# Decay attention, MLP and gated convolution in one kernel: order of loads, weight casts and the mixed input xr

## The chip, the cores and the metric

The kernel runs on one core of a Trainium2 chip. The metric is device time in microseconds (us) of one launch. TensorE (PE) multiplies matrices, VectorE (DVE), ScalarE (ACT) and GpSimd (POOL) do the elementwise work, and the queue of SyncE (SP) issues the loads and stores. Each engine works through its own queue in the order in which it was written; semaphores tie the queues together.

## The reference

Two batches, 768 tokens, model width 512, MLP width 1024, all float32. Three parts follow each other.

```python
# 1. attention with decay, 8 heads of width 64, state carried from block to block
intra = (q k^T * Dmask) v;   inter = (q * lam_pow) kv_state
out = intra + inter;         kv_state = lam_block * kv_state + (k * rev_pow)^T v
# 2. MLP on x and the token before it
xk = mu_k * x + (1 - mu_k) * x_prev;   xr = mu_r * x + (1 - mu_r) * x_prev
k = maximum(xk @ w_k, 0);   v = k * k @ w_v;   r = sigmoid(xr @ w_r);   x = r * v
# 3. gated convolution, 5 taps
gate = sigmoid(sum over taps of conv_w[j] * x shifted by 4 - j)
y = (gate * (x @ w_val)) @ w_out
```

## The kernel before

**Attention** goes over 12 chunks of 128 tokens (NCH = 12, six for each batch), all heads of a chunk at once. For chunk n TensorE does `scores(n)`, `update(n)` (the new state's product, not for the last chunk of a batch), `inter(n)` (not for the first chunk of a batch) and `attend(n)`. `scores(n + 1)` stands in front of `update(n)`. VectorE weighs the scores with the decay mask (`weigh`, two operations of 512 columns, L460) and adds the state (`new_state`, L474 and L477). GpSimd makes `kdec`, `qd` and `faded`. ScalarE copies the result out of PSUM into x (`evacuate_x`, L297), and `inter(n)` and `attend(n)` wait for the eviction of chunk n - 1, since they reuse its two banks.

Before it, TensorE does 24 dummy products (L781, WARM; each is two instructions in the trace), and VectorE makes the decay masks and `om` = 1 - mu from the small tensor `prm` (L546 to L552).

**Loads.** SP issues them all, in one written order (L198 to L218): `prm`, chunks 0 to 3, then weights and chunks mixed. A chunk is two tiles of 512 KB, qk and kv; it goes to one of four buffers, so `load_chunk(n)` waits for `att_done` of chunk n - 4, and what stands behind it on SP waits too. A weight piece is one tile of 512 KB: four for w_k, two for w_r, four for w_v. The four pieces of w2 (w_val and w_out) are issued when the last hidden product is done, into the place of w_k.

**Splitting.** Every operand of the MLP and the projections is split into a high part, cast to fp32r by ScalarE (`high`, `mix_high`, `kk_high`, L303, L320, L330), and a low part, the subtraction of the high part from the original, on VectorE (`low`, `mix_low`, `kk_low`, L495, L490, L504) or, for w_r and w_v, on GpSimd (L275). A product of k tiles is then three matmuls for each (L638, L639, L640): high by high, high by low, low by high.

**The MLP** goes over three tiles of 512 tokens (NT = 3, t = 0, 1, 2). For a tile TensorE does eight hidden products (`hidden(t, n)`, 12 matmuls of 512 columns each), four of receptance (`receptance(t, m)`, 12 each) and four value products (`value(t, m)`, 24 each). After each hidden product ScalarE does the relu (L326), VectorE the square (L499), then both split kk. `mix_part` (ScalarE, L314) and `mix` (VectorE, L484) build xk and xr. In each tile xr is built between its own hidden products: on ScalarE and VectorE alike one of its four steps stands with every second hidden product, the last high and low behind product 7. xk of the next tile is built during receptance. `new_x2` (L509) multiplies value and sigmoid, and writes in place into x.

What the order rests on: `hidden(0, 0)` waits for all of xk, w_k, the evictions of all 12 chunks, the weighing and the last state; `receptance(t, 0)` waits for all four `xr_l` of its tile and for w_r; `value(t, 0)` waits for all eight `kk_l` and for w_v; `hidden(t + 1, n)` with n of 4 or more waits for `new_x2(t, n - 4)`.

After the three tiles follow `val`, the taps of the convolution on VectorE (48 operations, L523), the gates and `project`, with stores of 256 KB each.

## Time and profile before

| | |
|---|---|
| median of 3 runs | 307.41 us (306.47 to 308.93) |
| the profiled execution | 305.9 us, of it span 304.0 us |
| TensorE busy | 286.8 us (94%) |
| VectorE, ScalarE, GpSimd busy | 164.6, 118.8, 48.1 us |
| mean granted clock of TensorE | 0.983 |
| HBM read, written | 20.01 MB, 3.15 MB |

The span runs from the first to the last instruction; the rest of the time lies around it. All times below are us from the start of the span. Attention fills the span up to 53, the three tiles of the MLP lie between 53 and about 234, and the rest follows.

### The profile page before, as it was taken

The numbers are of one execution on the slowest core, as the hardware profiler recorded it, in microseconds if no ns is written. First come the engines' busy times: TensorE is split into PE (matmuls) and PEld (weight loads), VectorE is DVE, ScalarE is ACT, GpSimd is POOL, SyncE is SP. The second block draws the span as 40 slices with busy tenths as digits, with TensorE's granted clock in tenths as the row PEclk, the third lists the DMA queues.
The fourth block names the chain that finished last, engine by engine and source line by source line (L and its number), as shares of the span: only waits on it lengthen the run. The fifth ranks groups of instructions, "written<-read, shape, count | busy, mean of one in ns | idle before, by whom it ended". The sixth has DMA issues, their size and how long they took to land.

```text
span 304.0 us, 4295 instructions
## 1 busy us (share of the span) xinstructions
PE 286.8 (94%) x1772; PEld 232.6 (77%) x1772; DVE 164.6 (54%) x251; ACT 118.8 (39%) x197; POOL 48.1 (16%) x38
## 2 busy tenths in 40 slices
PE   8998698999699999996999999789999999999996
PEld 8877586787488878875888888568887888887885
DVE  6547895298442004765444676621996879714100
ACT  1017624755362104645510155644711711612221
POOL 1684799950000000000000000000000000000000
PEclk9999899999799999999999999979999999999999
DMA  7999993000000000000000000070000000110122
GB/s 274 378 412 409 410 375 110 2 0 3 0 0 0 2 0 0 0 2 0 0 0 2 0 1 0 15 263 2 0 0 2 0 0 0 71 69 0 69 106 104
DMA packets 7506, 23.42 MB, mean 77 GB/s; under 512 B 832, under 2 KB 1216, under 8 KB 7488
## 3 DMA queue, kind: packets, MB, share of 16 engines
q1 hardware_dynamic: 7488, 23.16, 20.1%
q8 instruction: 14, 0.23, 0.3%
q14 instruction: 4, 0.03, 0.0%
HBM read 20.01 MB, written 3.15 MB: 76 GB/s over the span
## 4 chain that ended last, share of the span: by engine, by line
PE 90%; DVE 4%; DMA 3%; ACT 2%; issue 1%
PE ps L638 27%; PE ps L640 26%; PE ps L639 26%; PE ps L654 3%; PE ps L703 3%; DMA qk<-in_qk 3%; PE ps L781 2%; PE ps L671 1%; PE ps L688 1%; DVE xk_f L484 1%; DVE kk_f L499 1%; DVE pT L460 1%; DVE xr_l L490 1%; ACT ring L326 1%; DVE kk_l L504 1%
## 5 line engine op out<-in xcount | busy, mean ns | idle before, releaser
L638 PE MATMUL ps<-xk_h,wk_h 128*128 128x512 f32 x96 | 38.1, 397 | 0.8 <-issue 0.8
L639 PE MATMUL ps<-xk_l,wk_h 128*128 128x512 f32 x96 | 38.1, 396 | 0.0
L640 PE MATMUL ps<-kk_h,wv_l 128*128 128x512 f32 x96 | 38.1, 396 | 0.0
L638 PE MATMUL ps<-kk_h,wv_h 128*128 128x512 f32 x96 | 38.1, 396 | 0.0
L640 PE MATMUL ps<-xk_h,wk_l 128*128 128x512 f32 x96 | 38.0, 396 | 0.0
L639 PE MATMUL ps<-kk_l,wv_h 128*128 128x512 f32 x96 | 38.0, 396 | 0.0
L523 DVE SCALAR_TENSOR_TENSOR gate<-x,prm,gate 128x512 f32<-128x512 f32 x48 | 32.6, 746 | 0.0
L343 ACT ACTIVATE gate<-x,prm 128x512 f32<-128x512 f32 x12 | 8.7, 725 | 54.1 <-DVE x L509 54.1
L638 PE MATMUL ps<-xr_h,wr_h 128*128 128x512 f32 x48 | 20.7, 430 | 7.8 <-DVE xr_l L490 7.8
L499 DVE SCALAR_TENSOR_TENSOR kk_f<-ps,ring 128x512 f32<-128x512 f32 x24 | 16.5, 689 | 18.8 <-ACT ring L326 18.8
L509 DVE TENSOR_TENSOR x<-ps,r 128x512 f32<-128x512 f32 x12 | 8.3, 691 | 33.0 <-PE ps L640 33.0
L326 ACT ACTIVATE ring<-ps 128x512 f32<-128x512 f32 x24 | 14.3, 597 | 27.1 <-PE ps L640 27.1
L638 PEld LDWEIGHTS ps<-xk_h,wk_h 128*128 128x128 f32 x96 | 18.1, 188 | 5.4 <-issue 1.1
L639 PEld LDWEIGHTS ps<-kk_l,wv_h 128*128 128x128 f32 x96 | 18.1, 188 | 4.4
L640 PEld LDWEIGHTS ps<-kk_h,wv_l 128*128 128x128 f32 x96 | 18.1, 188 | 4.4
L640 PEld LDWEIGHTS ps<-xk_h,wk_l 128*128 128x128 f32 x96 | 18.1, 188 | 4.4
L638 PEld LDWEIGHTS ps<-kk_h,wv_h 128*128 128x128 f32 x96 | 18.1, 188 | 4.4
L639 PEld LDWEIGHTS ps<-xk_l,wk_h 128*128 128x128 f32 x96 | 18.1, 188 | 4.4
L460 DVE TENSOR_TENSOR pT<-ps,dec 128x512 f32<-128x512 f32 x24 | 15.3, 683 | 10.3 <-PE ps L654 10.2
L640 PE MATMUL ps<-xr_h,wr_l 128*128 128x512 f32 x48 | 20.2, 421 | 0.0
L639 PE MATMUL ps<-xr_l,wr_h 128*128 128x512 f32 x48 | 20.2, 421 | 0.0
L640 PE MATMUL ps<-w_h,gl 128*128 128x512 f32 (+1 forms) x52 | 19.8, 380 | 0.0
(69 smaller groups left out, 525.1 us busy)
## 6 DMA issues: line engine op xcount, KB each, us to landing
qk<-in_qk SPq DMA_DIRECT2D x12, 512.0 KB, 7.0
kv<-in_kv SPq DMA_DIRECT2D x12, 512.0 KB, 7.9
out<-out_sb SPq DMA_DIRECT2D x11, 256.0 KB, 2.0
wk_raw<-in_w_k SPq DMA_DIRECT2D x4, 512.0 KB, 10.1
wv_raw<-in_w_v SPq DMA_DIRECT2D x4, 512.0 KB, 8.7
wr_raw<-in_w_r SPq DMA_DIRECT2D x2, 512.0 KB, 8.5
w_raw<-in_w_val SPq DMA_DIRECT2D x2, 512.0 KB, 4.5
w_raw<-in_w_out SPq DMA_DIRECT2D x2, 512.0 KB, 8.0
```

The source lines that it names most:

```text
L326: nc.scalar.activation(ring[:, n % 4, :], ps[:, bank_of("mlp", t, n), :], ACT.Relu).then_inc(relu_ready, 1)
L343: nc.scalar.activation(like(t, gate[t][:, k, :]), x_cols(t, k, HALO), ACT.Copy, scale=prm[:, col:col + 1]).then_inc(tap0, 1)
L460: nc.vector.tensor_tensor(pT[:, n % 2, row, :], ps_s[n % 2][row], dec[:, row * PAIRS:(row + 1) * PAIRS, :].rearrange("p a i -> p (a i)"), ...
L499: nc.vector.scalar_tensor_tensor(out=kk_f[:, n, :], in0=ps[:, bank_of("mlp", t, n), :], scalar=0.0, in1=ring[:, n % 4, :], op0=ALU.max, op ...
L509: nc.vector.tensor_tensor(x_cols(t, m, 1), like(t, ps[:, bank_of("mlp", t, FT + KT + m), :]), like(t, r[:, m, :]), ALU.mult).then_inc(x2_r ...
L523: nc.vector.scalar_tensor_tensor(out=like(t, gate[t][:, k, :]), in0=x_cols(t, k, HALO - j), scalar=prm[:, col:col + 1], in1=like(t, gate[t ...
L638: nc.tensor.matmul(to, left(0), right(0), start=(i == 0), stop=False)
L639: nc.tensor.matmul(to, left(0), right(1), start=False, stop=False)
L640: done = nc.tensor.matmul(to, left(1), right(0), start=False, stop=(i == last))
L654: last = nc.tensor.matmul(ps_s[n % 2][row][:, cols], qk[i][rows_of(row), 1, cols], qk[i][rows_of(row), 0, cols], start=True, stop=True)
L703: last = nc.tensor.matmul(place_of(row, a), kv[i][:, 1, h * D:(h + 1) * D], pT[:, n % 2, row, a * P:(a + 1) * P], start=(c == 0 and a % 2 ...
L781: nc.tensor.matmul(ps[:, 7, 0:P], warm[:, :], warm[:, :], start=True, stop=True)
```

## The change

- `WARM` is 12 instead of 24.
- `prm` is issued by ScalarE, as its first instruction, and no more by SP.
- On SP only w_k's first piece stands ahead of chunk 4; the other weights move behind later chunks, all four pieces of w_v behind the last chunk.
- ScalarE: each weight cast of the attention stage but the first stands behind a later eviction than before (`wk_h` 1 behind that of chunk 5, `wk_h` 2 behind 7, `wk_h` 3 behind 8, `wr_h` 0 and 1 behind 9 and 10), and `wk_h` 0 behind that of chunk 2 instead of 3; the mixes of xk move a little. w_v is cast (`high`) behind hidden products 4 to 7 of tile 0.
- VectorE subtracts w_r (`low`) in place of GpSimd, and its steps on w_k and xk stand with other chunks. GpSimd keeps w_v.
- xr: for tile 0 the parts and mixes stand behind the last chunk, the high and low parts with hidden products 0 to 3. For tiles 1 and 2 all of it stands behind the receptance of the tile before.
- TensorE asks for all evictions at `hidden(0, 4)` and for the last state at `hidden(0, 6)`, instead of both at `hidden(0, 0)`.

```diff
-WARM = 24
+WARM = 12
@@ SP
-            sp.dma_start(prm[:, :], prm_in).then_inc(prm_here, 16)
             for n in range(IN_BUFS):
                 load_chunk(n)
             load_weight(wk_raw, w_k, 0, wk_here)
+            load_chunk(4)
             load_weight(wk_raw, w_k, 1, wk_here)
-            load_chunk(4)
+            load_chunk(5)
+            load_chunk(6)
             load_weight(wk_raw, w_k, 2, wk_here)
-            load_chunk(5)
+            load_chunk(7)
+            load_chunk(8)
             load_weight(wk_raw, w_k, 3, wk_here)
-            load_chunk(6)
-            load_chunk(7)
+            load_chunk(9)
+            load_chunk(10)
             load_weight(wr_raw, w_r, 0, wr_here)
-            load_chunk(8)
+            load_chunk(11)
             load_weight(wr_raw, w_r, 1, wr_here)
...
+            for i in range(4):
+                load_weight(wv_raw, w_v, i, wv_here)
@@ GpSimd
-            for i in range(2):
-                low(wr, wr_raw, i, wr_hi, wr_lo)
@@ ScalarE
+            act.dma_start(prm[:, :], prm_in).then_inc(prm_here, 16)
...
             evacuate_x(2)
+            high(wk, wk_raw, 0, wk_here, wk_hi)
             evacuate_x(3)
...
+            evacuate_x(5)
             high(wk, wk_raw, 1, wk_here, wk_hi)
-            evacuate_x(5)
+            mix_high(0, 2, 0)
+            mix_high(0, 3, 0)
+            evacuate_x(6)
+            evacuate_x(7)
             high(wk, wk_raw, 2, wk_here, wk_hi)
-            evacuate_x(6)
+            evacuate_x(8)
             high(wk, wk_raw, 3, wk_here, wk_hi)
-            evacuate_x(7)
-            evacuate_x(8)
+            evacuate_x(9)
             high(wr, wr_raw, 0, wr_here, wr_hi)
-            evacuate_x(9)
+            evacuate_x(10)
             high(wr, wr_raw, 1, wr_here, wr_hi)
-            evacuate_x(10)
-            high(wv, wv_raw, 0, wv_here, wv_hi)
             evacuate_x(11)
-            for i in range(1, 4):
-                high(wv, wv_raw, i, wv_here, wv_hi)
+            for k in range(KT):
+                mix_part(0, k, 1)
             for t in range(NT):
                 for n in range(FT):
-                    if n % 2 == 0:
-                        mix_part(t, n // 2, 1)
+                    if t == 0 and n < KT:
+                        mix_high(t, n, 1)
                     relu(t, n)
                     if n > 0:
                         kk_high(t, n - 1)
-                    if n % 2 == 1:
-                        mix_high(t, n // 2, 1)
+                    if t == 0 and n >= KT:
+                        high(wv, wv_raw, n - KT, wv_here, wv_hi)
...
+                if t + 1 < NT:
+                    for k in range(KT):
+                        mix_part(t + 1, k, 1)
+                    for k in range(KT):
+                        mix_high(t + 1, k, 1)
@@ VectorE
+                if n == 3:
+                    low(wk, wk_raw, 0, wk_hi, wk_lo)
                 if n == 4:
-                    low(wk, wk_raw, 0, wk_hi, wk_lo)
                     mix(0, 0, 0)
                     mix(0, 1, 0)
                 if n == 5:
                     mix(0, 2, 0)
                     mix(0, 3, 0)
+                if n == 6:
+                    low(wk, wk_raw, 1, wk_hi, wk_lo)
+                if n == 7:
                     mix_low(0, 0, 0)
-                if n == 6:
                     mix_low(0, 1, 0)
+                if n == 8:
                     mix_low(0, 2, 0)
-                if n == 7:
                     mix_low(0, 3, 0)
-                    low(wk, wk_raw, 1, wk_hi, wk_lo)
-                if n == 8:
+                if n == 9:
                     low(wk, wk_raw, 2, wk_hi, wk_lo)
-                if n == 9:
+                if n == 10:
                     low(wk, wk_raw, 3, wk_hi, wk_lo)
+                if n == 11:
+                    low(wr, wr_raw, 0, wr_hi, wr_lo)
+            low(wr, wr_raw, 1, wr_hi, wr_lo)
+            for k in range(KT):
+                mix(0, k, 1)
             for t in range(NT):
                 for n in range(FT):
-                    if n % 2 == 0:
-                        mix(t, n // 2, 1)
                     square(t, n)
                     if n > 0:
                         kk_low(t, n - 1)
-                    if n % 2 == 1:
-                        mix_low(t, n // 2, 1)
+                    if t == 0 and n < KT:
+                        mix_low(t, n, 1)
...
+                if t + 1 < NT:
+                    for k in range(KT):
+                        mix(t + 1, k, 1)
+                    for k in range(KT):
+                        mix_low(t + 1, k, 1)
@@ TensorE, hidden(t, n)
-                        pe.wait_ge(x_ready, NCH)
                         pe.wait_ge(p_ready, 2 * NCH)
-                        pe.wait_ge(state_ready, updates(NCH - 1))
+                if t == 0 and n == 4:
+                    pe.wait_ge(x_ready, NCH)
+                if t == 0 and n == 6:
+                    pe.wait_ge(state_ready, updates(NCH - 1))
```

## Rows read from the trace of the kernel before

**Rows 1.** The page, chain that ended last: shares of the span by engine.

```profile
PE 90%; DVE 4%; DMA 3%; ACT 2%; issue 1%
```

**Rows 2.** Waits of PE: who waited for whom, total us, times, longest us.

```profile
PE ps L638 <- DVE xr_l L490: 7.8, 3, 2.6
```

**Rows 3.** Chain in order of time, around `receptance(0, 0)`: start us, us, what.

```profile
76.23 0.60 ACT ring L326
...
78.15 0.61 DVE xr_l L490
...
78.81 0.51 PE ps L638
```

**Rows 4.** Table by stretch: us, busy of each engine, PEclk, DMA share, GB/s.

```profile
34.00:40.00 6.00, 5.76 (x80) 5.02 (x80) 5.24 (x10) 2.57 (x4) 4.60 (x4) 0.72 1.02 404
...
78.81:91.69 12.88, 12.88 (x48) 10.26 (x49) 5.33 (x8) 5.36 (x10) 0.00 (x0) 0.87 0.00 0
139.45:150.79 11.34, 11.34 (x49) 9.14 (x49) 5.33 (x8) 5.36 (x10) 0.00 (x0) 1.00 0.00 0
198.54:211.39 12.85, 12.85 (x48) 10.28 (x49) 2.77 (x4) 4.96 (x10) 0.00 (x0) 0.87 0.39 138
```

**Rows 5.** Timeline of ACT, 32 to 34: start us, us, what [idle before <-releaser].

```profile
32.57 1.04 ACT L303 CAST wk_h<-wk_raw 128x1024 fp32r<-128x1024 f32 x1
33.52 0.58 ACT L297 COPY x<-ps 128x512 f32<-128x512 f32 x1
```

**Rows 6.** Timeline of PE, from `attend(6)` to the first hidden product.

```profile
34.24 1.09 PE L703 MATMUL ps<-pT,kv 128*64 128x128 f32 x16 [2.64 <-ACT x L297]
35.27 2.08 PE L654 MATMUL ps<-qk 64*128 64x128 f32 x16
...
43.42 1.16 PE L654 MATMUL ps<-qk 64*128 64x128 f32 x16
...
46.74 1.16 PE L654 MATMUL ps<-qk 64*128 64x128 f32 x16
...
50.93 0.67 PE L688 MATMUL ps<-qd,state 64*64 64x128 f32 x16 [0.78 <-ACT x L297]
...
53.47 0.48 PE L638 MATMUL ps<-xk_h,wk_h 128*128 128x512 f32 x1 [0.85 <-issue]
```

**Rows 7.** Timelines of PE, ACT and DVE, the first 12 us.

```profile
1.05 7.27 PE L781 MATMUL ps<-warm 128*128 128x128 f32 x48 [1.05 <-DVE warm L540]
...
0.73 1.28 ACT L377 ACT_TABLE_LOAD   x1 [0.73 <-PEq L845]
...
6.58 0.96 DVE L552 TENSOR_SCALAR om<-prm 128x8 f32<-128x8 f32 x1
9.56 2.48 DVE L460 TENSOR_TENSOR pT<-ps,dec 128x512 f32<-128x512 f32 x4 [2.02 <-PE ps L654]
```

**Rows 8.** SP's issues of qk 1, 4, 11; under each, size and us to landing.

```profile
2.11 0.43 SPq L192 DMA_DIRECT2D qk<-in_qk  x1
qk<-in_qk SPq DMA_DIRECT2D x1, 512.0 KB, 5.7
...
12.13 0.33 SPq L192 DMA_DIRECT2D qk<-in_qk  x1
qk<-in_qk SPq DMA_DIRECT2D x1, 512.0 KB, 7.2
...
40.20 0.33 SPq L192 DMA_DIRECT2D qk<-in_qk  x1
qk<-in_qk SPq DMA_DIRECT2D x1, 512.0 KB, 4.8
```

**Rows 9.** Hidden products of tile 0: POOL and mix by line; one `kk_l` on DVE's timeline.

```profile
L275 POOL TENSOR_TENSOR wv_l<-wv_raw,wv_h 128x1024 fp32r<-128x1024 f32 x4 | 10.4, 2633 | 0.0
...
L484 DVE SCALAR_TENSOR_TENSOR xr_f<-x,om,xr_f 128x512 f32<-128x512 f32 x4 | 3.0, 745 | 7.0 <-ACT xr_f L314 7.0
...
60.60 2.08 DVE L504 TENSOR_TENSOR kk_l<-kk_f,kk_h 128x512 fp32r<-128x512 f32 x1
```

More of the change, by code:

```diff
@@ L201, in _ @@
             load_weight(wk_raw, w_k, 0, wk_here)
+            load_chunk(4)
             load_weight(wk_raw, w_k, 1, wk_here)
-            load_chunk(4)
+            load_chunk(5)
+            load_chunk(6)
             load_weight(wk_raw, w_k, 2, wk_here)
-            load_chunk(5)
+            load_chunk(7)
+            load_chunk(8)
             load_weight(wk_raw, w_k, 3, wk_here)
-            load_chunk(6)
-            load_chunk(7)
+            load_chunk(9)
+            load_chunk(10)
             load_weight(wr_raw, w_r, 0, wr_here)
-            load_chunk(8)
+            load_chunk(11)
             load_weight(wr_raw, w_r, 1, wr_here)
-            load_chunk(9)
-            load_weight(wv_raw, w_v, 0, wv_here)
-            load_chunk(10)
-            load_weight(wv_raw, w_v, 1, wv_here)
-            load_chunk(11)
-            load_weight(wv_raw, w_v, 2, wv_here)
-            load_weight(wv_raw, w_v, 3, wv_here)
+            for i in range(4):
+                load_weight(wv_raw, w_v, i, wv_here)
             sp.wait_ge(h_done, FT * NT)
@@ L380, in _ @@
             evacuate_x(2)
+            high(wk, wk_raw, 0, wk_here, wk_hi)
             evacuate_x(3)
-            act.wait_ge(om_ok, 1)
-            high(wk, wk_raw, 0, wk_here, wk_hi)
-            for k in range(KT):
+            for k in range(3):
                 mix_part(0, k, 0)
             evacuate_x(4)
-            for k in range(KT):
-                mix_high(0, k, 0)
-            high(wk, wk_raw, 1, wk_here, wk_hi)
-            evacuate_x(5)
-            high(wk, wk_raw, 2, wk_here, wk_hi)
-            evacuate_x(6)
-            high(wk, wk_raw, 3, wk_here, wk_hi)
-            evacuate_x(7)
-            evacuate_x(8)
-            high(wr, wr_raw, 0, wr_here, wr_hi)
-            evacuate_x(9)
-            high(wr, wr_raw, 1, wr_here, wr_hi)
-            evacuate_x(10)
-            high(wv, wv_raw, 0, wv_here, wv_hi)
-            evacuate_x(11)
-            for i in range(1, 4):
-                high(wv, wv_raw, i, wv_here, wv_hi)
+            mix_part(0, 3, 0)
+            mix_high(0, 0, 0)
+            mix_high(0, 1, 0)
+            evacuate_x(5)
+            high(wk, wk_raw, 1, wk_here, wk_hi)
+            mix_high(0, 2, 0)
+            mix_high(0, 3, 0)
+            evacuate_x(6)
+            evacuate_x(7)
+            high(wk, wk_raw, 2, wk_here, wk_hi)
+            evacuate_x(8)
+            high(wk, wk_raw, 3, wk_here, wk_hi)
+            evacuate_x(9)
+            high(wr, wr_raw, 0, wr_here, wr_hi)
+            evacuate_x(10)
+            high(wr, wr_raw, 1, wr_here, wr_hi)
+            evacuate_x(11)
+            for k in range(KT):
+                mix_part(0, k, 1)
             for t in range(NT):
                 for n in range(FT):
-                    if n % 2 == 0:
-                        mix_part(t, n // 2, 1)
+                    if t == 0 and n < KT:
+                        mix_high(t, n, 1)
                     relu(t, n)
```

## Prediction

> **What bounds the kernel now.** I began with the chain of work that ended last: TensorE holds 90% of it [rows 1], so a change pays where it closes a gap of TensorE, or where its clock was low. The table of waits names the gaps: three of 2.6 us in front of `receptance(t, 0)`, one for each tile t, all ending with `xr_l` from VectorE [rows 2]. The fourth gap of that size, 2.64 us, is in the attention stage and ends with ScalarE's eviction of x [rows 6]. The chain around the first kind shows why it is there [rows 3]: hidden products end at 76.2, and only then come relu (76.23), square, `kk_l`, and the last `xr_l`, which stands behind them in VectorE's order; the products with xr start at 78.81. The reader is to see that nothing in xr depends on the relu: only the order of the queue puts it there. The table of stretches adds the clock: the 48 receptance products take 12.88 and 12.85 us for tiles 0 and 2 (granted clock 0.87), and 11.34 for tile 1 (clock 1.00) after the same gap [rows 4]. In the attention stage ScalarE's queue explains the other gap: `wk_h` (L303) at 32.57 stands in front of the eviction at 33.52 [rows 5], and `attend(6)` waits for it until 34.24; the next scores then take 2.08 us where later ones take 1.16 [rows 6]. The clock of 34 to 40 is 0.72 [rows 4]. Loads run at full share and 404 GB/s meanwhile (last columns of that row): attention is close to a second bound, the DMA engines.
>
> **The attention stage, step by step.**
> *Start.* TensorE's 48 dummy matmuls take 7.27 us from 1.05 [rows 7]. Without half of them the row ends near 4.7 by the mean, later if the first ones are slow. `scores(0)` takes 1.1, then `scores(1)` waits for chunk 1's qk: it was issued at 2.11 and took 5.7, so 7.8 [rows 8]; with `prm` (0.43 us of SP's time, 84 KB) off SP's queue about 7.4. So dummies could end as late as 6.3 and cost nothing; that needs the removed 24 to be worth 2 us, 83 ns each, where the mean is 151. VectorE is the other input: its constants end at 6.58 + 0.96 = 7.54, yet it began to weigh at 9.56, held by scores [rows 7]. Now it weighs chunk 0 from 7.6 to 8.8; TensorE does scores(1) to 8.5, the update (0.6) to 9.1, attends (1.03) to 10.15. Before, attend(0) ended at 12.08. The start is 1.9 us earlier.
> `prm` is issued by ScalarE. If its table load of 1.28 us (0.73 [rows 7]) goes first, the constants and attend(0) are up to 1.3 late; if not, nothing. I take nothing, since the start has slack against the loads below.
> *Pace.* Without a wait a chunk takes 3.32 us: 43.42 to 46.74 [rows 6] (scores 1.09, update 0.61, inter 0.60, attend 1.03). Chunks 5 and 6 lack one part each, 2.7. Loads go in the order of the SP queue: chunk 4's qk is the 11th tile of 512 KB and landed at 12.13 + 7.2 = 19.33, chunk 11's qk the 31st, landed at 40.20 + 4.8 = 45.0 [rows 8]. That is 1.284 us per tile. The new order makes the qk of chunks 4 to 11 tiles number 10, 13, 15, 18, 20, 23, 25 and 28. From 18.9 for tile 11 (0.43 less) they land at 17.6, 21.5, 24.0, 27.9, 30.5, 34.3, 36.9, 40.7. Scores of the next chunk go in front of each attend, so attend(n) ends at the later of attend(n-1) and the landing of qk n+1, plus the chunk's time: 10.15, 13.5, 16.8, 20.9, 24.8, 27.55, 30.6, 34.0, 37.6, 41.0, 44.3. The waits for loads add up to about 1.9 us (0.8, 0.6, 0.35, 0.3 and less). Chunk 11 has no scores in front: it waits 0.78 for the eviction of chunk 10, as now [rows 6], and ends at 46.7; now it ends at 52.6.
> ScalarE no longer stands in front of its evictions: `wk_h` 1, 2 and 3 are called after evictions at 26, 34 and 37.6, and their tiles (12, 17, 22) land at 20, 27 and 33. `wr_h` 1 (tile 30, 43.3) is called after eviction 10 at 44.3. So the 2.64 us gap goes, and the slow clock after it: scores 0.92, update and inter about 0.6, 1.5 us [rows 6].
> *VectorE.* With its steps moved it has, per chunk, 1.7 us of weighing and state, and one weight subtraction (up to 2 us) or two mixes (1.4). From chunk 6 on it is about full; with the subtraction at 2 us its last `wk_l` ends at 46.3 (weighing of chunk 11 from 42.7, state 10 at 44.3). Hidden products need that and no longer the last eviction (asked for only at n = 4, and the last state at n = 6). So the 0.85 us in front of the first of them [rows 6] becomes 0.1 to 0.2: first hidden product at 46.9 instead of 53.47, 6.6 us earlier. This term is bounded below by the loads without the early slack (first attend at 11.4, clock low once more, VectorE 1 us late): 4; above, if the loads catch up with the chunks and only the 3.33 us pace is left: 8.
>
> **The three tiles.** xr of tile 0 is built by ScalarE and VectorE at the start of its hidden products; `wr_l` goes from GpSimd to VectorE (two operations; even at GpSimd's 2.6 us each they end some 20 us before receptance wants them), `wv_h` and `wv_l` behind hidden products 4 to 7. xr of tiles 1 and 2 is built during the value products of the tile before. Those are 96 matmuls, as the hidden ones, which take 22.7 us from 53.47 to 76.2 [rows 3, 6]. Four parts and four high on ScalarE, four mixes and four low on VectorE, at no more than the mix's 745 ns each [rows 9], are under 6 us on either engine, and done some 8 us after receptance. `new_x2(t, 0)` stands behind them on VectorE; its product ends 5.6 us into the stage, so it comes 2 us late, and next in line is value product 1 at 11.2: caught up by then. Nothing on TensorE waits for `x` before the hidden product 4 of the next tile. So receptance can follow hidden products at once, and this takes 2.61 plus 0.1 of slower first issue each: 3 x 2.7 = 8.1 us. The low clock after the gap of tiles 0 and 2 goes with its cause: 12.88 + 12.85 - 2 x 11.34 = 3.1 us [rows 4]. It could be as little as 0, if the clock falls at other places; I take 3.1, since no stretch without a gap of over 2 us ahead of it shows less than full clock.
> What is late next: `value(t, 0)` asks for all `kk_l`. Receptance covers it with 11.3 us; the last `kk_l` is ready some 4 us after the hidden products (in [rows 3] the order behind 76.2 is relu, square, `kk_l`, `xr_l`, all by 78.8; one more round for product 7). In tile 0 it also asks for `wv_l`.
> GpSimd's four `wv_l` take 10.4 us, now from about 61 on instead of 54.5; while it works, a `kk_l` subtraction ran 2.08 us instead of 0.68 [rows 9]. The Trainium skill (SBUF — State Buffer, on the shared port pair) says that a VectorE operation with two SBUF inputs and a GpSimd operation exclude each other for the whole instruction; the row agrees, with its 2.08. By it each of the `kk_l` of products 4 to 7 may wait out a GpSimd operation. By the row: `wv_h` 3 is ready 2.1 us after the hidden products, `wv_l` 3 takes 2.6, and a `kk_l` blocked behind it ends after some 6, and the value products start after 11.3. Cost nothing with 5 us of cover. Without the cover it would be those 6 us.
> The tail (val, gates, project) hangs on the end of receptance of tile 2, with the same work behind it as before, so it moves as a block. Only the w2 loads don't: they start with the end of hidden products, and have 12.4 us instead of 16.4 until ScalarE wants them, against a landing within 9.
>
> **Sum.** 6.6 + 8.1 + 3.1 = 17.8 us. The profiled span is 304.0, so 286.2; with the 1.9 us around it (305.9) 288.1. The three runs have a median of 307.41, 1.5 above the profiled one, which would give 289.6. I take 289.0, between them.
>
> **Rivals.**
> *Loads or VectorE hold attention, or the clock falls once more* (15 in 100). For it: loads already run without a pause, and VectorE is full from chunk 6 on. Then the first term is 4 or less, and one or two low stretches of 1.55 stay: 292 to 296.
> *The receptance wait becomes a wait of the value products or of hidden product 4* (6 in 100), through GpSimd's share of VectorE's time. Against it are 5 us of cover. One such wait would give 3 to 6 us back, in tile 0 alone: 292 to 295.
> *Slower than before* (3 in 100). One mechanism: with 12 dummies and a pause between scores(0) and scores(1), TensorE gets the low clock for attention. Chunk time would go from 3.3 to up to 6.6, and it decides from the sixth slow chunk on (17.8 / 3.3 = 5.4); with all twelve the time would be 289 + 12 x 3.3 = 329 us. Against it: the pause is under 1.5 us, and TensorE had three waits of about 0.5 us in attention at full clock; the half clock stood in this trace only behind 2.6 us of pause [rows 4, 6].
> The Trainium skill (TensorE: Matmul & The Clock Gate, Part 1) says that warming up is a matter of busy time and not of the number of matmuls. By that rule halving `WARM` could leave scores slow; scores(0) would then take 2 us instead of 1.1 and still end before 7.4.
> *The change does nothing in the tiles* (2 in 100): if some other input of receptance were as late as `xr_l`. `wr_l` and the square of product m are long done in the rows, so this is unlikely: 300.
>
> **Chances.** The forecast itself has 74 in 100, its own range 286 to 292 (first term 4 to 8, clock 0 to 3.1 and the 1.5 between profile and median). With the rivals next to it the range is 285 to 295. A measurement of this kernel can tell about 1% from no change. All cases but the slow clock end more than 1% faster (the fourth barely): faster 0.95, same 0.02, slower 0.03.
>
> **What would show it.** Right: the receptance matmuls follow the hidden ones with no idle time in all three tiles; each receptance stretch is 11.3 us at clock 1.00; the first L638 starts near 47; the wait for ScalarE's x in front of `attend` is gone but for 0.8 at the end; waits for qk of 0.3 to 0.8 us at chunks 4, 5, 7 and 9. Wrong: the first hidden product after 49, a wait for `wk_l`, `kk_l` or `wv_l`, or a granted clock under 0.9 in some stretch.

## The result, and the profile after

| | before | after |
|---|---|---|
| median | 306.94 us (304.76 to 308.93, 4 runs) | 289.84 us (289.81 to 290.29, 4 runs) |
| ratio | | 0.9447, 95% interval 0.9405 to 0.949 |
| profiled execution, its span | 305.9, 304.0 us | 289.8, 287.9 us |
| first hidden product starts at | 53.47 | 49.01 |
| from there to the end of the span | 250.5 | 238.9 |

The changed kernel takes 289.84 us where 289.0 was forecast, 17.1 us less than before. The waits of TensorE come first (who waited for whom, total, times, longest; line numbers are those of the changed kernel, in which L650 to L652 are the three matmuls of a product, L715 attends, L666 are scores, L683 updates and L700 inter):

```profile
PE ps L715 <- DVE pT L462: 1.8, 1, 1.8
PE ps L666 <- DMA qk<-in_qk: 1.3, 2, 0.8
PE ps L795 <- DVE warm L542: 1.1, 1, 1.1
PE ps L683 <- issue: 0.9, 1, 0.9
PE ps L700 <- ACT x L292: 0.8, 1, 0.8
PE ps L683 <- POOL kdec L253: 0.3, 1, 0.3
```

The line of [rows 2] has no counterpart: no product waits for `xr_l`. TensorE's timeline at the end of the hidden products of tile 0 shows what stands where 2.61 us of idle time stood [rows 3]: the first L650 on `xr_h` follows 0.23 us behind the last L652 on `xk_h`.

```profile
71.37 0.39 PE L652 MATMUL ps<-xk_h,wk_l 128*128 128x512 f32 x1
71.60 0.40 PE L650 MATMUL ps<-xr_h,wr_h 128*128 128x512 f32 x1
...
82.61 0.39 PE L652 MATMUL ps<-xr_h,wr_l 128*128 128x512 f32 x1
82.85 0.39 PE L650 MATMUL ps<-kk_h,wv_h 128*128 128x512 f32 x1
```

From 71.60 to 82.85 are 11.25 us for the 48 receptance matmuls of tile 0, which took 12.88 in [rows 4]. The table of stretches (columns as in [rows 4]; the two halves of the span, then a stretch within each receptance) has the clock at 1.00 throughout in this execution:

```profile
0.00:49.00 49.00, 42.86 (x728) 36.54 (x728) 38.94 (x65) 18.25 (x27) 32.73 (x32) 1.00 0.94 367
49.00:288.00 239.00, 236.36 (x1022) 190.44 (x1020) 127.54 (x189) 100.41 (x170) 9.72 (x4) 1.00 0.06 23
...
71.60:82.90 11.30, 11.30 (x50) 9.09 (x49) 8.60 (x10) 8.46 (x14) 4.41 (x2) 1.00 0.00 0
128.00:139.00 11.00, 11.00 (x48) 8.85 (x48) 6.69 (x10) 7.44 (x13) 0.00 (x0) 1.00 0.01 1
184.00:195.00 11.00, 11.00 (x48) 8.84 (x48) 4.06 (x6) 6.92 (x13) 0.00 (x0) 1.00 0.57 193
```

The attention stage is where the forecast was off. The start did not move forward. `prm` on ScalarE's queue took 4.0 us to land, VectorE's constants began at 4.79, and the first attend at 11.20, where it had been 10.99. The first issue of SP and the one of ScalarE, 0.01 us apart (size, us to landing):

```profile
qk<-in_qk SPq DMA_DIRECT2D x1, 512.0 KB, 3.8
prm<-in_prm ACTq DMA_DIRECT2D x1, 84.0 KB, 4.0
```

VectorE's timeline, and TensorE's under it:

```profile
4.79 2.63 DVE L548 TENSOR_TENSOR_SCAN dec<-prm 128x128 f32<-128x128 f32 x8 [3.60 <-DMA prm<-in_prm]
...
9.77 2.48 DVE L462 TENSOR_TENSOR pT<-ps,dec 128x512 f32<-128x512 f32 x4 [0.20 <-DVE om L554]
```

```profile
11.20 1.09 PE L715 MATMUL ps<-pT,kv 128*64 128x128 f32 x16 [1.78 <-DVE pT L462]
```

Behind that the chunks run nearly without a wait, the 2.64 us and the low clock of [rows 4, 6] are gone, and what remains is loads (0.79 and 0.49 us, at chunks 8 and 9), one wait for `kdec` (GpSimd's `kdec` of chunk 10 ended at 44.20) and the last eviction:

```profile
31.70 1.16 PE L666 MATMUL ps<-qk 64*128 64x128 f32 x16 [0.79 <-DMA qk<-in_qk]
...
35.59 1.16 PE L666 MATMUL ps<-qk 64*128 64x128 f32 x16 [0.49 <-DMA qk<-in_qk]
...
44.30 0.69 PE L683 MATMUL ps<-kv,kdec 128*64 128x64 f32 x16 [0.87 <-issue]
...
47.39 0.67 PE L700 MATMUL ps<-qd,state 64*64 64x128 f32 x16 [0.78 <-ACT x L292]
...
49.01 0.50 PE L650 MATMUL ps<-xk_h,wk_h 128*128 128x512 f32 x1
```

### The profile page after: what moved, and what is told of

Same layout as the page of the kernel before. It is cut to its first block, busy times and chain, and to the rows that moved or that the text cites. A ratio compares the mean times of both kernels' runs of the same rounds, so it can differ in the third digit from the quotient of the medians.

```text
span 287.9 us, 4245 instructions
## 1 busy us (share of the span) xinstructions
PE 279.2 (97%) x1748; PEld 227.0 (79%) x1748; DVE 166.5 (58%) x253; ACT 118.7 (41%) x197; POOL 42.5 (15%) x36
## 4 chain that ended last, share of the span: by engine, by line
PE 92%; DMA 4%; DVE 2%; issue 1%; ACT 0%; DVEq 0%
PE ps L650 27%; PE ps L652 27%; PE ps L651 27%; PE ps L715 4%; PE ps L666 3%; DMA qk<-in_qk 2%; PE ps L700 2%; PE ps L683 2%; DMA prm<-in_prm 1%; DVE dec L548 1%; DVE qdec L552 1%; DVE pT L462 0%; ACT x L292 0%; ACT out_sb L368 0%; DVE om L554 0%
## 5 line engine op out<-in xcount | busy, mean ns | idle before, releaser
L650 PE MATMUL ps<-xk_h,wk_h 128*128 128x512 f32 x96 | 38.2, 397 | 0.0
L652 PE MATMUL ps<-xk_h,wk_l 128*128 128x512 f32 x96 | 38.1, 396 | 0.0
L652 PE MATMUL ps<-kk_h,wv_l 128*128 128x512 f32 x96 | 38.1, 396 | 0.0
L651 PE MATMUL ps<-kk_l,wv_h 128*128 128x512 f32 x96 | 38.1, 396 | 0.0
L651 PE MATMUL ps<-xk_l,wk_h 128*128 128x512 f32 x96 | 38.1, 396 | 0.0
L650 PE MATMUL ps<-kk_h,wv_h 128*128 128x512 f32 x96 | 38.1, 396 | 0.0
L501 DVE SCALAR_TENSOR_TENSOR kk_f<-ps,ring 128x512 f32<-128x512 f32 x24 | 16.6, 692 | 33.0 <-ACT ring L321 32.8
L650 PEld LDWEIGHTS ps<-xk_h,wk_h 128*128 128x128 f32 x96 | 18.1, 188 | 4.5 <-issue 0.2
L650 PEld LDWEIGHTS ps<-kk_h,wv_h 128*128 128x128 f32 x96 | 18.1, 188 | 4.4
L652 PEld LDWEIGHTS ps<-xk_h,wk_l 128*128 128x128 f32 x96 | 18.1, 188 | 4.4
L652 PEld LDWEIGHTS ps<-kk_h,wv_l 128*128 128x128 f32 x96 | 18.1, 188 | 4.4
L650 PE MATMUL ps<-w_h,gh 128*128 128x512 f32 (+1 forms) x52 | 19.8, 381 | 0.0
L652 PE MATMUL ps<-w_h,gl 128*128 128x512 f32 (+1 forms) x52 | 19.6, 376 | 0.0
L651 PE MATMUL ps<-w_l,gh 128*128 128x512 f32 (+1 forms) x52 | 19.5, 375 | 0.0
L292 ACT COPY x<-ps 128x512 f32<-128x512 f32 x12 | 7.1, 588 | 29.7 <-PE ps L715 29.7
L650 PE MATMUL ps<-x2h,w_h 128*128 128x512 f32 x48 | 19.0, 397 | 0.0
```

Of the source, the lines that this page charges most:

```text
L292: nc.scalar.copy(x[:, :, cols].rearrange("p (g a) i -> p g a i", g=2), ps[:, 4:6, 0:2 * CH].rearrange("p g (a i) -> p g a i", a=2)).then_i ...
L501: nc.vector.scalar_tensor_tensor(out=kk_f[:, n, :], in0=ps[:, bank_of("mlp", t, n), :], scalar=0.0, in1=ring[:, n % 4, :], op0=ALU.max, op ...
L650: nc.tensor.matmul(to, left(0), right(0), start=(i == 0), stop=False)
L651: nc.tensor.matmul(to, left(0), right(1), start=False, stop=False)
L652: done = nc.tensor.matmul(to, left(1), right(0), start=False, stop=(i == last))
```

## Experiments

Three groups of four kernels; each group shared the runs of the kernel before on its chip (medians 306.51, 305.86 and 306.46 us).

### The two halves apart: xr_only and attn_only

`xr_only` is the kernel before with the new places of xr:

```diff
+            for k in range(KT):
+                mix_part(0, k, 1)
...
                 for n in range(FT):
-                    if n % 2 == 0:
-                        mix_part(t, n // 2, 1)
+                    if t == 0 and n < KT:
+                        mix_high(t, n, 1)
                     relu(t, n)
...
-                    if n % 2 == 1:
-                        mix_high(t, n // 2, 1)
...
+                if t + 1 < NT:
+                    for k in range(KT):
+                        mix_part(t + 1, k, 1)
+                    for k in range(KT):
+                        mix_high(t + 1, k, 1)
```

and the same on VectorE. `...` stands for lines left out. `attn_only` is the changed kernel with these edits reversed.

> The kernel before with only the change of xr: for tile 0 its parts and mixes behind the last chunk and its high and low parts with hidden products 0 to 3, for tiles 1 and 2 all of it behind the receptance of the tile before. Loads, attention, weight casts and the 24 dummies are as before. Theory (the gap in front of receptance was only a place in VectorE's queue, and the low clock only its consequence): all three gaps of 2.7 us go and both low stretches of receptance (12.88 and 12.85 us) become 11.3, so 11.2 us less than before, about 295.7 us against 306.9, and this is more than two thirds of the whole gain. Rival (the low clock of tiles 0 and 2 has its own cause, such as the load of work before it): only 8.1 us less, 298.8, with a granted clock under 0.9 in some receptance stretch.

> The changed kernel with xr built as before, between the hidden products of its own tile; loads, attention stage, dummies, prm on ScalarE's queue and w_v's late casts as changed. Theory: the two halves of the change are independent, so this gives what xr_only does not, 4.5 us of the first hidden product (53.47 to 49.0) and the three gaps stay: about 302 us, with gaps of 2.6 us in front of receptance. Rival (the halves interact: GpSimd's late w_v subtractions now collide with xr's low parts in tile 0): the gap of tile 0 grows beyond 2.6 us, by up to one GpSimd operation of 2.4, and the time is 304 or more.

Measured: `xr_only` 295.62 us (294.31 to 296.32), ratio 0.9614 (0.957 to 0.9659). That is 10.9 us less than before, against 11.2 expected. TensorE has no gap behind the first hidden product, and from there to the end of the span are 238.8 us (55.57 to 294.4), as in the changed kernel, against 250.5 before. In the profile's row of 40 slices, shown under the first hidden product, the clock is low in attention alone, behind the gap of the eviction, which was 3.60 us in this execution:

```profile
55.57 0.47 PE L648 MATMUL ps<-xk_h,wk_h 128*128 128x512 f32 x1 [0.85 <-issue]
...
PEclk9999879999999999999999999999999999999999
```

Its rival asked for a low stretch in a receptance, and there is none. So the low clock of tiles 0 and 2 was a consequence of the gap, and the sum of the terms 8.1 and 3.1 stands. The 3.1 is a matter of the execution: a gap of 2.6 us was not followed by a low clock each time. It was in tiles 0 and 2 of the kernel before, and in tiles 0 and 1 of `attn_wv_early` below.

`attn_only` 308.11 us (306.30 to 308.96, 10 runs), ratio 1.003 (1.0001 to 1.006): no gain at all, where about 302 was expected. Its waits, the TensorE row at tile 0 (L640 is the first matmul of a product, L487 `xr_l`), and the stretch behind it:

```profile
PE ps L640 <- DVE xr_l L487: 11.7, 3, 6.5
```

```profile
80.86 0.80 PE L640 MATMUL ps<-xr_h,wr_h 128*128 128x512 f32 x1 [6.47 <-DVE xr_l L487]
```

```profile
80.86:94.00 13.14, 13.14 (x46) 10.47 (x47) 4.79 (x8) 5.19 (x9) 0.00 (x0) 0.79 0.00 1
```

The gap of tile 0 grew from 2.61 to 6.47 us, and receptance behind it took 13.8 us (80.86 to 94.64) at a clock of 0.79. VectorE's timeline, and GpSimd's under it, say why:

```profile
72.03 2.47 DVE L481 SCALAR_TENSOR_TENSOR xr_f<-x,om,xr_f 128x512 f32<-128x512 f32 x1 [0.35 <-ACT xr_f L309]
74.42 0.68 DVE L496 SCALAR_TENSOR_TENSOR kk_f<-ps,ring 128x512 f32<-128x512 f32 x1
75.03 2.23 DVE L501 TENSOR_TENSOR kk_l<-kk_f,kk_h 128x512 fp32r<-128x512 f32 x1
77.19 0.68 DVE L496 SCALAR_TENSOR_TENSOR kk_f<-ps,ring 128x512 f32<-128x512 f32 x1
77.79 2.41 DVE L501 TENSOR_TENSOR kk_l<-kk_f,kk_h 128x512 fp32r<-128x512 f32 x1
80.12 0.68 DVE L487 TENSOR_TENSOR xr_l<-xr_f,xr_h 128x512 fp32r<-128x512 f32 x1
```

```profile
71.45 5.26 POOL L272 TENSOR_TENSOR wv_l<-wv_raw,wv_h 128x1024 fp32r<-128x1024 f32 x2 [0.92 <-ACT wv_h L298]
77.30 2.35 POOL L272 TENSOR_TENSOR wv_l<-wv_raw,wv_h 128x1024 fp32r<-128x1024 f32 x1 [0.58 <-ACT wv_h L298]
```

Three VectorE operations with both inputs in SBUF (L481, L501 twice) take 2.2 to 2.5 us beside a GpSimd operation; the squares between them (L496), with one input in PSUM, take 0.68. The profiled span is 3.0 us longer than before: 1.8 less for the first hidden product (51.63), 3.9 more for the gap, 0.9 more for receptance. That the first hidden product came at 51.63, and not at 49.0 as expected, is the low clock of the section on the dummies below.

### Is it w_v on GpSimd? attn_wv_early

On top of `attn_only`:

```diff
             evacuate_x(11)
+            for i in range(4):
+                high(wv, wv_raw, i, wv_here, wv_hi)
...
-                    if t == 0 and n >= KT:
-                        high(wv, wv_raw, n - KT, wv_here, wv_hi)
```

> attn_only (xr built as before) with one more thing as before: ScalarE casts all of w_v right behind the last eviction, so that GpSimd's four subtractions run during hidden products 0 to 4 instead of 4 to 8. In attn_only the gap in front of receptance of tile 0 was 6.47 us, and a VectorE mix and two subtractions behind hidden products 5 to 7 took 2.2 to 2.5 us each instead of 0.7, each beside a GpSimd subtraction of w_v. Theory (VectorE and GpSimd keep each other out of SBUF, so late w_v work stretches the xr steps): the gap of tile 0 is 2.6 to 3.0 us again, those operations take 0.7 to 0.8, and the time is about 304, 3.5 to 4 less than attn_only's 308.1. Rival (the longer gap comes from ScalarE's w_v casts of 1.05 us standing in its queue, not from the lock; or from xr started later): with the casts in front of the whole tile ScalarE is late at its start, the gap stays above 4 us.

Measured: 303.08 us (302.26 to 304.04), ratio 0.9883 (0.9819 to 0.9947), against 308.1 and 1.003 of `attn_only` in the other group. All three gaps are 2.6 us (7.8 in total), and the `kk_l` and `xr_l` behind hidden products 5 to 7 take 0.68. The rival falls: ScalarE was late at the start of the tile (the first mix of xr waited for it until 56.71) and the gap was short all the same. This edit moves ScalarE's casts and GpSimd's subtractions together; that it is GpSimd's that count rests on the timeline above, where three VectorE operations take 5.0 us more than the 0.68 and 0.74 that the same operations take alone. So the late w_v work costs nothing in the changed kernel only because xr has left that part of the hidden loop. The move of w_v alone, without the rest of the attention half, was not run.

### Where prm is issued: prm_sp, prm_act_alone

```diff
+            sp.dma_start(prm[:, :], prm_in).then_inc(prm_here, 16)
             for n in range(IN_BUFS):
                 load_chunk(n)
...
-            act.dma_start(prm[:, :], prm_in).then_inc(prm_here, 16)
```

In `prm_act_alone` ScalarE still issues it, and SP begins with `sp.wait_ge(prm_here, 16)`.

> The changed kernel with prm issued first on SP's queue again, as before, not on ScalarE's. In the changed kernel prm landed 4.04 us after its issue instead of 2.0, VectorE's constants ended at 9.56 instead of 7.54 and attend(0) started at 11.20. Theory (prm's packets wait between those of the chunk loads when they come from another queue; and the late attend(0) issues chunk 4 late, so that the loads run dry for 1.2 us): prm lands in 2.0 us, attend(0) starts near 9.2, chunk 4's qk lands 0.8 to 1.2 us earlier, and the first hidden product starts 0.8 to 1.2 us earlier than 49.0: time about 289 against 289.8. Rival 1 (loads alone set the pace, the start has slack): attend(0) earlier, first hidden product unchanged or 0.4 later, 289.8 to 290.2. Rival 2 (prm would be late wherever it is issued, since chunk tiles start at the same time): prm still lands after about 4 us.

> The changed kernel, prm issued by ScalarE as there, but SP waits until it has landed before it issues the first chunk. Theory (prm lands after 4.0 us instead of 2.0 because its small packets take turns with the chunks' large ones): alone it lands after 1.9 to 2.1 us. Rival (ScalarE's queue itself is slow): still 4 us. All chunk loads are about 2 us late by construction, so the total, some 291, is not the question; the second question is the load rate between 12 and 32 us, which was 380 to 396 GB/s in the three kernels with prm on ScalarE and 405 to 413 without: if the use of the second queue alone lowers it, it stays near 385.

Measured: in `prm_act_alone` prm landed after 1.9 us, from the same queue of ScalarE that took 4.0 with chunk loads beside it. So the queue is not slow; company is. The mechanism of that company (turns between packets, as expected in words) is not shown, only that it costs 2 us. The load rate between 16 and 28 us was 411 GB/s, so using the second queue does not lower it by itself. The kernel was run once: 290.98 us.

`prm_sp` 289.36 us (288.97 to 290.09), ratio 0.9418 (0.938 to 0.9456). prm landed after 1.9, the first attend started at 9.66 instead of 11.20, chunk 4 was issued at 10.76 instead of 12.34, and the first hidden product started at 48.16 instead of 49.01: 0.85 earlier from a start 1.5 earlier. Its times overlap with those of the changed kernel (289.81 to 290.29): that it gains 0.85 us rests on the two profiles. Its waits for qk:

```profile
PE ps L666 <- DMA qk<-in_qk: 2.8, 5, 1.0
```

These five are the 1.0 in front of scores(1), and 0.47, 0.43, 0.41 and 0.57 at chunks 4, 5, 7 and 9: with a start 0.6 us from the one that the prediction had assumed (9.66 against 9.1), its list of waits comes true. Its rival 1 had half of it: the loads absorb about half of the earlier start.

### The dummies: warm24, and the group that settles the clock

`warm24` and `warm24_again` are the changed kernel with `WARM = 24`, `prm_sp_warm24` is `prm_sp` with it; `after_again` and `prm_sp_again` are repeats.

> The changed kernel with 24 dummy products instead of 12. Theory: in the changed kernel TensorE idled 1.78 us in front of attend(0) for VectorE's constants, so 12 more dummies (about 2.7 us at full clock) are nearly covered: attend(0) starts at 11.2 to 11.6 instead of 11.20, the loads absorb it, and the time is that of the changed kernel within 0.3 us. Rival (the halving was part of the gain at the start): 1 to 2 us slower than the changed kernel.

> The changed kernel once more, unaltered, as the reference of this group on the same chip. Theory: the time of its first measurement, 289.8 us within 0.5, and no granted clock under 0.95 in the attention stage. Rival (the attention stage of the changed kernel loses the clock in some executions, as in the profile of attn_only, where the same stage had a granted clock of 0.68 from 12 to 16 us and the first hidden product came at 51.6 instead of 49.0): some of its times 1.5 to 2.5 us above the others.

> The changed kernel (prm on ScalarE) with 24 dummies, a second time. Its first group gave 290.1 to 290.8 us with clock 1.00; the changed kernel with 12 gave 289.8 to 290.3 in one group and 290.6 to 292.4 in another, whose profile had the low clock behind attend(0). Theory (12 more dummies fill the wait in front of attend(0), so the clock never falls there): 290.0 to 290.8 again, all granted clocks above 0.95 in the attention stage. Rival (the fall does not depend on the dummies): some runs at 292 with a low stretch between 11 and 16 us.

> prm_sp once more, unaltered, as the reference of this group. The changed kernel itself differed between two groups (289.8 and 291.7 us), and in its second profile the clock was 0.60 from 12 to 16 us behind waits of 0.3, 0.4 and 1.8 us. Theory (with prm on SP no wait of that length stands in the attention stage, so that stage keeps the clock): 289.0 to 289.8 us again, spread under 1.3 us, granted clock 1.00 throughout. Rival (the difference between the groups is one of chips): it moves by about 2 us as well, to 291 or more, with the clock at 1.00.

> prm_sp with 24 dummy products instead of 12. Theory (with prm early, it is the dummies that hold scores(0), as in the kernel before): attend(0) starts near 11 instead of 9.66, chunk 4's loads are issued as late as in the changed kernel (12.1 to 12.3), and the first hidden product starts 0.5 to 1.2 us later than prm_sp's 48.2: 289.9 to 290.6. Rival (the loads absorb the start): within 0.2 us of prm_sp. It also tells what lowers the load rate between 16 and 28 us (299 to 392 GB/s in every kernel with prm on ScalarE beside the chunks, 405 to 413 in the others): if late issue of chunk 4 does, it is low here too; if prm's packets on a second queue at the start do, it is 405 or more.

| kernel | prm beside chunks on ACT's queue | dummies | times, us | clock 11 to 16 us | chunk 4 issued | GB/s 16 to 28 us |
|---|---|---|---|---|---|---|
| after | yes | 12 | 289.8 to 290.3 | 1.00 | 12.34 | 385 |
| after_again | yes | 12 | 290.6 to 292.4 | 0.66 | 12.75 | 320 |
| warm24 | yes | 24 | 290.1 to 290.8 | 1.00 | 12.57 | 373 |
| warm24_again | yes | 24 | 289.6 to 290.6 | 1.00 | 13.01 | 352 |
| prm_sp | no | 12 | 289.0 to 290.1 | 1.00 | 10.76 | 410 |
| prm_sp_again | no | 12 | 289.4 to 290.9 | 1.00 | 11.00 | 413 |
| prm_sp_warm24 | no | 24 | 289.5 to 290.9 | 1.00 | 12.60 | 373 |

`after_again` lost the clock in the stage in which the prediction's third rival put it. TensorE's waits up to attend(0), and the stretch behind it:

```profile
7.22 1.16 PE L666 MATMUL ps<-qk 64*128 64x128 f32 x16 [0.29 <-DMA qk<-in_qk]
8.74 0.69 PE L683 MATMUL ps<-kv,kdec 128*64 128x64 f32 x16 [0.36 <-POOL kdec L253]
11.21 1.49 PE L715 MATMUL ps<-pT,kv 128*64 128x128 f32 x16 [1.78 <-DVE pT L462]
```

```profile
12.00:16.00 4.00, 4.00 (x55) 3.29 (x52) 1.83 (x5) 0.59 (x1) 2.86 (x3) 0.60 1.02 384
```

A low clock followed: from the start of attend(0) to that of attend(1) are 4.87 us instead of 3.33, so 1.5 us lost. The first hidden product came at 51.26 instead of 49.01; the median is 291.70, ratio 0.9517 (0.9461 to 0.9574). The expectation, 289.8 within 0.5 and no low clock, failed, and its rival came true. Of the four profiles with 12 dummies and prm beside the chunks (after, `after_again`, `attn_only`, `attn_wv_early`, one attention stage in all) three have a clock of 0.66 from 11 to 16; of the two with 24 dummies none; of the six with prm landed in 2 us (`prm_sp` twice, `prm_sp_warm24`, `prm_act_alone`, and the two of the next section) none.

The mean clock of each execution, profiled or not, says the same. It is 0.994 in four of the eight executions of the changed kernel (290.29, 291.35, 292.06 and 292.44 us) and 1.000 in the other four (289.81 to 290.55). It is 1.000 in all eight with 24 dummies, and 0.999 or more in all 21 of the six kernels with prm landed in 2 us. So in the changed attention stage no execution fell without both, few dummies and a late prm; with both it depends on the execution.

Not all of the 1.9 us between `after` and `after_again` is the clock. `after_again` took 290.55 even at clock 1.000, the loads of its profile moved 320 GB/s where those of `after` moved 385, and `prm_sp_again` has a median 0.9 us above that of `prm_sp` at full clock, outside the 289.0 to 289.8 expected. So the medians of two groups can differ by 0.9 us for the same kernel at full clock.

`warm24` started attend(0) at 11.43, as expected, and its median of 290.47 is 0.6 us above that of the changed kernel, where 0.3 was the expected bound and 1 to 2 the rival's; groups alone differ by more than that. `warm24_again` came out as expected, at 290.35 us (289.58 to 290.56) and full clock. The dummies taken out are worth nothing that shows: `prm_sp_warm24` has 290.07 us against 290.26 of `prm_sp_again` beside it, with its first attend at 11.46 instead of 9.91 and its first hidden product at 49.04 instead of 48.60. In the time the rival of its expectation, that the loads absorb the start, holds.

The last column answers the question on the rate. Chunk 4 late in the new order of loads (12.29 or more) gives 320 to 385 GB/s, with prm on either queue (321 and 335 in `attn_wv_early` and `attn_only`); at 11.6 or less it is 410 to 413. The old order with two weight pieces ahead of chunk 4 keeps 412 at 12.13 [rows 8] and 411 at 13.16 (`xr_only`). From 12 to 32 us the two sets stay apart as well, 392 to 407 against 349 to 387. So a low rate goes with a late chunk 4 that has only one weight piece ahead of it. That the loads run dry there is an inference: in `after_again` the DMA share falls to 0.62 between 18 and 19 us, but in the changed kernel it is 1.01 from 16 to 28 at the lower rate. The low spell stands in 16 to 20 us of `prm_sp_warm24`, and in the changed kernel is spread up to 28; why it spreads stays open:

```profile
16.00:20.00 4.00, 4.00 (x78) 3.47 (x78) 1.62 (x3) 1.26 (x3) 3.91 (x5) 1.00 0.94 293
20.00:28.00 8.00, 8.00 (x160) 6.64 (x158) 6.69 (x11) 5.42 (x9) 5.42 (x5) 1.00 1.03 413
```

### The gate of the first hidden product: waits_back

On top of `prm_sp`:

```diff
-                if t == 0 and n == 4:
+                if t == 0 and n == 0:
                     pe.wait_ge(x_ready, NCH)
-                if t == 0 and n == 6:
                     pe.wait_ge(state_ready, updates(NCH - 1))
```

> prm_sp with the waits for all evictions and for the last state back at hidden(0, 0), as in the kernel before, instead of at hidden(0, 4) and (0, 6). Theory (the last eviction lands about 0.65 us behind the last attend): TensorE idles 0.8 to 0.9 us in front of the first hidden product, as the 0.85 us of before, and the time is 0.8 us above prm_sp's. Rival (the last wk_l on VectorE, which is full there, ends as late as the last eviction): less than 0.3 us difference.

```profile
50.10 0.47 PE L650 MATMUL ps<-xk_h,wk_h 128*128 128x512 f32 x1 [0.89 <-ACT x L293]
```

The wait of 0.89 us is there, as the 0.85 of [rows 6]; VectorE's last `wk_l` had ended at 47.23, so it did not bind. In the time it can't be told: 290.54 us (289.29 to 290.88) against 290.26 (289.38 to 290.86) of `prm_sp_again`, where 0.8 more was expected. Without the 0.89 us the first hidden product of this profile would still start at 49.21, behind longer waits for qk (3.8 us in total, the longest 1.56 and 1.43).

### A version beyond both: loads_late

```diff
             load_weight(wk_raw, w_k, 0, wk_here)
-            load_weight(wk_raw, w_k, 1, wk_here)
             load_chunk(4)
             load_chunk(5)
+            load_weight(wk_raw, w_k, 1, wk_here)
             load_chunk(6)
-            load_weight(wk_raw, w_k, 2, wk_here)
             load_chunk(7)
+            load_weight(wk_raw, w_k, 2, wk_here)
...
-            load_weight(wk_raw, w_k, 3, wk_here)
             load_chunk(9)
             load_chunk(10)
-            load_weight(wr_raw, w_r, 0, wr_here)
+            load_weight(wk_raw, w_k, 3, wk_here)
             load_chunk(11)
+            load_weight(wr_raw, w_r, 0, wr_here)
```

This stands on top of `prm_sp`, and on GpSimd `decay_k(n + 1)` ahead of `decay_q(n + 1)` from chunk 9 on.

> prm_sp (prm on SP) with two more moves. On SP the pieces of w_k come one or two chunks later (piece 0 behind chunk 3, 1 behind chunk 5, 2 behind 7, 3 behind 10) and w_r behind chunk 11, so that the qk of chunks 5, 7, 9, 10 and 11 is one 512 KB tile (1.28 us) further ahead; on GpSimd kdec of chunks 9 and 10 is made before qd of the same chunk, since update comes before inter. Theory (the chunk loads bind at chunks 4 to 9, and kdec of chunk 10 held TensorE for 0.8 us): waits for qk after chunk 4 vanish or halve, the kdec wait goes, the first hidden product starts 1.3 to 2.0 us earlier than prm_sp's 48.16, and the time is 287.4 to 288.1. Rival (weights landing later hold the last wk_l on VectorE, or TensorE's own 3.33 us per chunk binds): first hidden product within 0.5 us of 48.2, 289.4.

Measured: 288.56 us (288.31 to 289.31), ratio 0.9422 (0.9371 to 0.9474), beside 290.55 to 292.44 of `after_again` in the same group: its times don't overlap the changed kernel's there. It has the lowest median of all, but missed the 287.4 to 288.1 expected, and relative to the kernel before in its own group it is no better than `prm_sp` (0.9422 against 0.9418). The first hidden product starts at 47.65, 0.5 before that of `prm_sp`, less than the 1.3 expected. The wait for `kdec` is gone and one for `qd` of the same size has taken its place (timelines of TensorE, VectorE and GpSimd):

```profile
43.56 0.67 PE L703 MATMUL ps<-qd,state 64*64 64x128 f32 x16 [0.78 <-POOL qd L266]
```

```profile
41.15 1.21 DVE L500 TENSOR_TENSOR wk_l<-wk_raw,wk_h 128x1024 fp32r<-128x1024 f32 x1
```

```profile
41.16 2.34 POOL L266 TENSOR_TENSOR qd<-qk,qdec 128x512 f32<-128x512 f32 x1
```

GpSimd's `qd` of 1.27 us took 2.34 behind VectorE's `wk_l`, which started 0.01 us before it. GpSimd works from 33.8 to 45.3 us without a pause here, as it does from 31.9 to 46.0 in the changed kernel. So at the end of attention it looks like the bound, and its order only chooses which product waits; a kernel with less work on GpSimd was not run.

## Why the prediction came out as it did

The time was within 0.8 us of the forecast and inside the range, but one of the prediction's own signs of being wrong came up: the first hidden product started after 49, at 49.01 and in `after_again` at 51.26. By its steps:

- **Gap in front of receptance, 8.1 us.** Right: no wait in all three tiles, and `xr_only` isolates it.
- **Low clock behind the gaps, 3.1 us.** Right, with the same kernel: 10.9 of 11.2 us for the two terms together. Each alone was not measured in the time; in the profile the receptance of tile 0 went from 12.88 to 11.25 us.
- **First hidden product, 6.6 us.** Wrong in size: 4.5 in the profiled execution (49.01), and 2.2 in that of `after_again` (51.26). The start and GpSimd failed, and the loads in part.
  - *Start, 1.9 us.* The prediction asked only whether ScalarE's table load might go first (it does not: issued at 0.73, the load follows at 1.16) and let VectorE's constants end at 7.54 as before, that is, it took prm's landing time of 2.0 us along to the other queue. It was 4.0. The 24 dummies left took 5.06 us, where the mean of before had given 3.6; they held nothing up. The start came to nothing, attend(0) at 11.20 against 10.99 before and 9.1 forecast. As foreseen, the loads absorbed part: `prm_sp` puts the start right and is 0.85 us earlier at the first hidden product.
  - *Loads.* The count of tiles at 1.284 us held: forecast 17.6, 21.5, 24.0 and 27.9 for the qk of chunks 4 to 7, measured 17.4, 21.3, 23.9 and 27.7. From chunk 8 on all are 1.2 to 1.3 us late (31.7, 35.6, 38.1, 42.0 against 30.5, 34.3, 36.9, 40.7), after a low rate from 16 to 28 us, which goes with the late issue of chunk 4. With prm on SP's queue (`prm_sp`) all eight land within 0.5 us of the forecast.
  - *GpSimd.* The wait of 0.87 us for `kdec` of chunk 10 was not in the list. The prediction counted VectorE's load per chunk (1.7 + 2) and not GpSimd's (1.06 + 0.62 + 1.27 and the time for which VectorE's subtractions keep it out), though it had named that exclusion for the tiles.
  
  Together: from the start of attend(0) to the first hidden product are 37.8 us, as forecast (9.1 to 46.9). In them the waits for loads are 1.3 us instead of 1.9, since the late start gave the loads time, and `kdec`'s 0.9 stands in place of the rest. So in this execution the miss of 2.1 us is the late start. A right start would not have saved all of it: `prm_sp` has one and is still 1.3 us late at the first hidden product, of which 0.56 lies ahead of its attend(0) and 0.77 is its wait for `kdec`.
- **The 0.85 us gate.** Right: hidden follows attend at once, and `waits_back` brings back 0.89.
- **The rival of GpSimd and the value products.** The cover held: the last `kk_l` was ready at 77.5, value products began at 82.85. One mix took 2.42 us beside GpSimd's last subtraction. The mechanism was rated at 6 in 100 and rightly did not decide, but `attn_only` shows that it lengthens the gap by 3.9 us, from 2.6 to 6.47, where the cover is absent. The Trainium skill's rule (SBUF — State Buffer, on the shared port pair) agrees with these rows in both directions: VectorE's 0.7 becomes up to 2.5, GpSimd's 1.27 becomes 2.34, and squares, with one of two inputs in PSUM, stay at 0.68.
- **The slow clock in attention.** The prediction held it for the rare way to a slower kernel, through all twelve chunks. It happened, in three profiles of four of this attention stage, for one chunk and a half. The price was 0.5 to 1.9 us and not 40, by the executions of one group at mean clock 0.994 against those at 1.000. The pause between scores(0) and scores(1) is not needed for it: it was 0.29, 0.47 and none in the three. The 1.8 us in front of attend(0), prm's doing, stood in all three, but in the first profile without a fall as well.
- **The sum.** The span was forecast as 286.2 and is 287.9: 2.1 us late at the first hidden product, and 0.4 less than forecast behind it. The offset of 0.9 us towards the median hid half of that. So that the time came as close as 0.8 us is partly luck: by mechanism the forecast was 2.1 us off in the attention stage.

## What to carry to other kernels

When an engine waits at a stage border, look at what stands in the releasing engine's queue behind work of the stage that ends there: here the last xr step had no need of the relu in front of it, and moving it into a stage in which VectorE idles gave 10.9 of 17 us. Test two moves apart as well as together: the second half of this change gains nothing alone (308.1 against 306.5), since its late w_v work on GpSimd stretches the very steps that the first half moves away. A small tensor on which a whole stage waits belongs in front of the large loads, on the same queue: here it landed 2 us earlier so. In the time that showed as 0.5 us (`prm_sp`), which is within what groups differ by.

## What the runs showed of the hardware that was not expected

- An 84 KB load issued at the same moment as 512 KB loads from another queue landed after 3.9 to 4.0 us in six kernels and 1.8 to 2.0 us when issued first on the same queue, or alone on the other.
- The clock fell behind a wait of 1.8 us at 11 us, with one or two of 0.3 to 0.5 us ahead of it, in three profiles of four. The waits for qk in `waits_back`, 1.56 us at 6.4 and 1.43 us at 20.9, did not lower it.
- The same 48 dummy matmuls (24 products) took 7.27 us in the kernel before, and 8.30, 7.71, 7.74 and 8.14 in others with the same loop; the 24 of the shorter loop took 4.29 to 5.49. No run here tells what sets that.
